# A second attention product on 64x64 tiles in two banks, with the transposes in one of them

## The reference

```python
for c in range(nc):                       # 24 chunks of 32, 4 batches, 8 heads, head size 64
    scores = scale * q_c @ k_full.T       # 32 x 64
    a = np.exp(scores - max);  a = a / (sum(a) + 1e-9)
    out[c] = a @ v_full                   # the second attention product
# x = heads side by side
h = x @ w_in;  e = np.exp(h - max);  solu = h * e / (sum(e) + 1e-9)
ln = (solu - mean) / sqrt(var + 1e-6) * g_ln
y = ln @ w_out                            # 3072 x 512
g = np.maximum(0.01 * (y @ w_in2), y @ w_in2);  out = g @ w_out2
```

## Time and profile before

| | us |
|---|---|
| median of three runs (lowest, highest) | 807.08 (806.21, 808.84) |
| the profiled execution | 806.93 |
| its span, first to last instruction | 805.1 |
| busy: PE, PEld, DVE, ACT, POOL | 793.7, 652.5, 542.0, 454.7, 62.6 |
| mean granted TensorE clock | 0.999 of full speed |
| one `expo`, 128x384 | 0.52 |
| one `rsum`: sum, addition, reciprocal | 0.55, 0.18, 0.19 |
| one `probs` on GpSimd | 0.83 |
| one `x_lo` (xT_lo), 128x384 | 0.55 |
| one `solu`: product, read of the sum, mean | 1.21, 0.08, 0.15 |
| one `expo1`, one `norm`, one `tr`, 128x1024 | 1.11, 1.24, 1.22 |

### The profile page before, as it was taken

The page is one execution under the profiler, slowest core; times in us unless marked ns, Lnnn a source line. Parts: engine busy times, 40 slices in busy tenths (PEclk is TensorE's granted clock), DMA queues, the critical chain, the costliest instruction groups (busy, mean ns, idle before and its releaser), DMA issues.

```text
span 805.1 us, 14444 instructions
## 1 busy us (share of the span) xinstructions
PE 793.7 (99%) x5604; PEld 652.5 (81%) x5604; DVE 542.0 (67%) x902; ACT 454.7 (56%) x737; POOL 62.6 (8%) x156
## 2 busy tenths in 40 slices
PE   8989999999999999999999999999999999999998
PEld 6778888888888888888888888888888888888886
DVE  6788889987632556436652335756799698779774
ACT  5578877777543345256574447666644555445553
POOL 1233332332100000000000000000000000000000
PEclk9999999999999999999999999999999999999999
DMA  9855878755938975167684567545933740462002
GB/s 357 290 173 199 254 242 249 220 163 138 303 93 274 319 270 210 52 209 248 224 285 158 202 234 244 171 166 174 375 135 102 264 158 26 140 245 113 27 1 78
DMA packets 79891, 156.72 MB, mean 195 GB/s; under 512 B 6224, under 2 KB 30928, under 8 KB 79824
## 3 DMA queue, kind: packets, MB, share of 16 engines
q1 hardware_dynamic: 79824, 155.81, 57.4%
HBM read 99.16 MB, written 56.62 MB: 193 GB/s over the span
## 4 chain that ended last, share of the span: by engine, by line
PE 92%; DVE 4%; DMA 2%; issue 1%; ACT 1%; SPq 0%; POOL 0%; DVEq 0%; ACTq 0%
PE hid_a L731 23%; PE hid_b L731 21%; PE scores_ps L731 21%; PE attn_ps L731 13%; PE probs_ps L731 7%; PE attn_ps L723 3%; PE scores_ps L697 2%; DMA g_scratch<-g_out 1%; PE probs_ps L709 1%; DVE ring_lo L1147 1%; DVE g_blk L1289 0%; DMA attn_buf<-qk_in 0%; DVE unit_max L1165 0%; DVE g_blk L1294 0%; DVE shifted L1168 0%
## 5 line engine op out<-in xcount | busy, mean ns | idle before, releaser
L862 ACT ACTIVATE ring_hi<-g_blk 128x512 fp32r<-128x512 f32 x168 | 105.8, 632 | 108.2 <-PE hid_b L731 40.1
L1147 DVE TENSOR_TENSOR ring_lo<-g_blk,ring_hi 128x512 fp32r<-128x512 f32 x168 | 115.6, 688 | 38.4 <-ACT ring_hi L862 35.3
L1011 ACT ACTIVATE g_out<-g_out 128x512 f32<-128x512 f32 x72 | 45.4, 630 | 71.3 <-DVE g_out L1273 41.1
L731 PE MATMUL scores_ps<-x_op_P_hi,w_hi 128*128 128x512 f32 x144 | 56.1, 390 | 0.0
L731 PE MATMUL scores_ps<-x_op_P_lo,w_hi 128*128 128x512 f32 x144 | 56.0, 389 | 0.0
L731 PE MATMUL scores_ps<-x_op_P_hi,w_lo 128*128 128x512 f32 x144 | 56.0, 389 | 0.0
L731 PE MATMUL hid_b<-ring_hi,w_hi 128*128 128x512 f32 x128 | 50.0, 391 | 0.2 <-DVE ring_lo L1147 0.2
L731 PE MATMUL hid_b<-ring_lo,w_hi 128*128 128x512 f32 x128 | 49.9, 390 | 0.0
L731 PE MATMUL hid_b<-ring_hi,w_lo 128*128 128x512 f32 x128 | 49.8, 389 | 0.0
L731 PE MATMUL hid_a<-w_in_hi,xT_hi 128*128 128x512 f32 x96 | 39.6, 412 | 1.0 <-DVE xT_lo L1147 0.9
L1147 DVE TENSOR_TENSOR w_lo<-w_raw,w_hi 128x1792 fp32r<-128x1792 f32 (+2 forms) x24 | 33.6, 1401 | 8.4 <-ACT w_hi L862 8.2
(11 more groups left out here) (178 smaller groups left out, 2043.7 us busy)
## 6 DMA issues: line engine op xcount, KB each, us to landing
g_scratch<-g_out SPq DMA_DIRECT2D x96, 256.0 KB, 2.7
g_blk<-g_scratch SPq DMA_DIRECT2D x48, 512.0 KB, 7.3
attn_buf<-qk_in SPq DMA_DIRECT2D x32, 576.0 KB, 6.5
attn_buf<-v_in SPq DMA_DIRECT2D x32, 384.0 KB, 3.9
ln_scratch<-lnT SPq DMA_DIRECT2D x24, 512.0 KB, 6.3
w_raw<-w_in SPq DMA_DIRECT2D x16, 512.0 KB, 4.4
ln_even<-ln_scratch SPq DMA_DIRECT2D x12, 512.0 KB, 6.6
ln_odd<-ln_scratch SPq DMA_DIRECT2D x12, 512.0 KB, 7.2
```

What stands on the lines that cost most here:

```text
L731: mm = pe.matmul(psum, weights[i], data[j], start=first and n == 0, stop=last and n == 2, skip_group_check=goes_on)
L862: return act.activation(dst, src, ACT.Copy)
L1011: act.activation(x, x, ACT.Prelu, alpha=0.01).then_inc(s_g[q], 1)
L1147: return ve.tensor_tensor(dst, x, hi.bitcast(f32), ALU.subtract)
```

## The change

- `values` becomes 24 products on 64x64 tiles (64 rows by 64 columns of weights, 32 columns of data, straight from the transposed probabilities `prob_t`). The two row halves write to two banks, `attn_ps[:, 0:512]` and `attn_ps[:, 512:]`.
- `spread` becomes one copy of 128x384 from PSUM into `prob_t`; `diag` with its memsets is gone.
- `probs_ps` is gone: the transposes write into the first bank of `attn_ps`. So `probs_t` of a unit waits for `x_lo` of the unit before instead of for `spread`.
- `x_hi` and `x_lo` read the two banks and write every second run of 32 tokens, through a four-dimensional view.
- The list of steps is written anew: `probs_t` and `values` of the same unit now follow each other with one slice of `hidden` between them; in BLOCK_STEPS T of 4t+3, H, V of 4t+3, S of 4t+6. START and TAIL are reordered likewise.

```diff
 START, from its fifth line:
+        ("values", 1), ("load_v", 5), ("probs", 2), ("x_hi", 1), ("x_lo", 1),
+        ("scores", 3), ("load_qk", 7), ("w1_lo", 1),
+        ("hidden", 1, 0), ("shift", 3), ("w1_hi", 2),
+        ("probs_t", 2), ("spread", 2), ("expo", 3),
+        ("hidden", 0, 1), ("w1_lo", 2), ("rsum", 3), ("w1_hi", 3), ("probs", 3),
+        ("values", 2), ("load_v", 6), ("x_hi", 2), ("x_lo", 2),
+        ("hidden", 1, 1), ("w1_lo", 3),
+        ("hidden", 0, 2),
+        ("probs_t", 3), ("spread", 3),
+        ("hidden", 1, 2),
+        ("values", 3), ("load_v", 7), ("x_hi", 3), ("x_lo", 3),
+        ("scores", 4), ("load_qk", 8), ("shift", 4), ("expo", 4), ("rsum", 4), ("probs", 4),
+        ("hidden", 0, 3),
+        ("scores", 5), ("load_qk", 9), ("shift", 5), ("neg_max", 0), ("expo", 5),
+        ("hidden", 1, 3), ("expo1", 0), ("rsum", 5), ("probs", 5),
+        ("probs_t", 4), ("stats_a", 0), ("spread", 4), ("solu", 0),
+        ("scores", 6), ("load_qk", 10), ("square", 0), ("neg_max", 1),
+        ("values", 4), ("load_v", 8), ("stats", 0), ("x_hi", 4), ("x_lo", 4),
+        ("hidden", 2, 0), ("shift", 6), ("expo1", 1), ("expo", 6), ("rsum", 6), ("probs", 6), ("stats_a", 1),
+        ("probs_t", 5), ("spread", 5), ("solu", 1), ("norm", 0),
+        ("hidden", 2, 1), ("square", 1), ("tr", 0),
+        ("values", 5), ("load_v", 9), ("x_hi", 5), ("x_lo", 5),
+        ("scores", 7), ("load_qk", 11), ("shift", 7), ("expo", 7), ("rsum", 7), ("probs", 7),
+        ("hidden", 2, 2),
+        ("scores", 8), ("load_qk", 12), ("shift", 8), ("expo", 8), ("rsum", 8), ("probs", 8),
+        ("probs_t", 6), ("spread", 6),
+        ("values", 6), ("load_v", 10),
 BLOCK_STEPS, its middle:
+        ("probs_t", 4), ("spread", 4), ("norm", -1), ("w1_lo", 2),
+        ("hidden", 0, 3), ("neg_max", 0),
+        ("values", 4), ("load_v", 8), ("x_hi", 4), ("x_lo", 4),
+        ("scores", 7), ("load_qk", 11), ("expo1", 0), ("shift", 7), ("stats_a", 0),
+        ("hidden", 1, 1), ("expo", 7), ("solu", 0),
+        ("hidden", 1, 2), ("rsum", 7), ("probs", 7),
...
 def probs_t(a):
                 if a >= 1:
-                    pe.wait_ge(s_spread, 2 * a)
+                    pe.wait_ge(s_x_lo, a)
...
             def values(a):
                 pe.wait_ge(s_v_in[a % SLOTS], 16 * (a // SLOTS + 1))
-                pe.wait_ge(s_spread, 2 * (a + 1))
-                if a >= 1:
-                    pe.wait_ge(s_x_lo, a)
+                pe.wait_ge(s_spread, a + 1)
+                buf, pt = attn_buf[a % SLOTS], prob_t[a % 2]
+                for pair in range(BLOCK_CHUNKS // 2):
+                    for r in range(2):
+                        rows = slice(ROWS * r, ROWS * r + ROWS)
                         for hb in range(2):
+                            n = 2 * pair + hb
+                            first = BLOCK + SEG + n * HEAD_DIM
+                            mm = pe.matmul(attn_ps[64 * hb:64 * hb + 64, HALF * r + CHUNK * pair:HALF * r + CHUNK * (pair + 1)],
+                                           buf[rows, first:first + HEAD_DIM],
+                                           pt[rows, n * CHUNK:(n + 1) * CHUNK], start=True, stop=True)
                 mm.then_inc(s_values, 1)
...
             def spread(a):
-                for half in range(2):
-                    rows = slice(64 * half, 64 * half + 64)
-                    copy(diag[a % 2][rows, :, half, :],
-                         probs_ps[rows, 0:BLOCK].rearrange("k (n q) -> k n q", q=CHUNK)).then_inc(s_spread, 1)
+                copy(prob_t[a % 2][:, :], attn_ps[:, 0:BLOCK]).then_inc(s_spread, 1)
...
             def x_hi(a):
-                copy(xT[t % 2][0][:, hp, :], attn_ps[:, 0:BLOCK]).then_inc(s_x_hi, 1)
+                copy(of_halves(xT[t % 2][0][:, hp, :]), attn_halves).then_inc(s_x_hi, 1)
...
-            for i in range(2):
-                ve.memset(diag[i][:, :, :, :], 0.0).then_inc(s_init, 1)
```

More of the change, by code:

```diff
@@ L118 @@
         ("hidden", 0, 0), ("expo", 2), ("w1_hi", 1), ("rsum", 2),
[L119 to L143, removed]
@@ L170 @@
-        ("hidden", 2, 2), ("rsum", 8), ("square", 1),
-        ("probs_t", 7),
-        ("values", 6), ("load_v", 10), ("tr", 0), ("probs", 8), ("w1_hi", 3),
+        ("scores", 5), ("load_qk", 9), ("x_hi", 2), ("x_lo", 2), ("stats", -2),
+        ("hidden", -1, 3), ("norm", -2), ("shift", 5),
+        ("hidden", 0, 0), ("expo", 5), ("neg_max", -1), ("rsum", 5), ("probs", 5),
+        ("probs_t", 3), ("spread", 3),
+        ("hidden", 0, 1), ("expo1", -1), ("tr", -2), ("solu", -1), ("stats_a", -1),
@@ new lines @@
+        ("values", 3), ("load_v", 7), ("x_hi", 3), ("x_lo", 3),
+        ("scores", 6), ("load_qk", 10), ("square", -1), ("shift", 6),
+        ("hidden", 0, 2), ("expo", 6), ("stats", -1),
+        ("hidden", 1, 0), ("rsum", 6), ("probs", 6),
+        ("probs_t", 4), ("spread", 4), ("norm", -1), ("w1_lo", 2),
+        ("hidden", 0, 3), ("neg_max", 0),
+        ("values", 4), ("load_v", 8), ("x_hi", 4), ("x_lo", 4),
+        ("scores", 7), ("load_qk", 11), ("expo1", 0), ("shift", 7), ("stats_a", 0),
@@ new lines @@
+        ("hidden", 1, 1), ("expo", 7), ("solu", 0),
+        ("hidden", 1, 2), ("rsum", 7), ("probs", 7),
+        ("probs_t", 5), ("spread", 5), ("square", 0), ("tr", -1),
+        ("hidden", 1, 3), ("neg_max", 1), ("stats", 0),
+        ("values", 5), ("load_v", 9), ("x_hi", 5), ("x_lo", 5),
+        ("scores", 8), ("load_qk", 12), ("norm", 0), ("shift", 8),
+        ("hidden", 2, 0), ("expo1", 1), ("stats_a", 1), ("expo", 8),
+        ("hidden", 2, 1), ("solu", 1),
+        ("probs_t", 6), ("spread", 6), ("square", 1), ("rsum", 8), ("probs", 8),
@@ L173 @@
+        ("hidden", 2, 2), ("tr", 0), ("w1_hi", 3),
+        ("values", 6), ("load_v", 10),
 )
 TAIL = (
-        ("hidden", 20, 3), ("x_hi", 30), ("stats", 19), ("spread", 31), ("x_lo", 30),
+        ("hidden", 20, 3), ("x_hi", 30), ("stats", 19), ("x_lo", 30),
         ("hidden", 21, 0), ("neg_max", 20), ("norm", 19),
+        ("probs_t", 31), ("spread", 31),
         ("hidden", 21, 1), ("expo1", 20), ("tr", 19),
@@ L322, in build @@
     prob = [at(f"prob{i}", (77 + 1.5 * i) * KB, [P, BLOCK]) for i in range(2)]
-    diag = [at(f"diag{i}", (112 + 3 * i) * KB, [P, BLOCK // P * 4, 2, CHUNK]) for i in range(2)]
+    prob_t = [at(f"prob_t{i}", (112 + 1.5 * i) * KB, [P, BLOCK]) for i in range(2)]
     xT = [[at(f"xT{i}_{x}", (place + 6 * j) * KB, [P, KM, BLOCK], f32r) for j, x in enumerate(("hi", "lo"))]
@@ L1183, in x_lo @@
                 ve.wait_ge(s_x_hi, a + 1)
-                rest(xT[t % 2][1][:, hp, :], attn_ps[:, 0:BLOCK], xT[t % 2][0][:, hp, :]).then_inc(s_x_lo, 1)
+                rest(of_halves(xT[t % 2][1][:, hp, :]), attn_halves, of_halves(xT[t % 2][0][:, hp, :])).then_inc(s_x_lo, 1)
             def neg_max_(n):
```

25 lines of the change are left out of this document (8 added, 17 removed).

## The result

The changed kernel takes 821.2 us (median of 4 runs, 820.5 to 825.0) against 806.9 for the kernel before on the same chip: ratio 1.018, 95% interval 1.015 to 1.022. It is slower by 14 us, where 4 were forecast and 816 was the upper end of the range. Its mean granted clock is 0.987; the other three executions show 0.990 to 0.992, so the share of the clock in the sum is that of this execution.

The account below looks back on a forecast made before the run. TensorE, busy 99% of the span, was taken to bound the kernel. Its own work -0.2, regular part +0.3 and START's waits +3.7 gave +3.8 us on 807.1, so 810.9 us; range 808.0 to 816.0.

Parts of the forecast that it names:

- Direction and mechanism: Whole kernel: slower, chance 0.78, with idle time in START before PE steps waiting for spread, x_lo and shift.
- PE's own work, -0.2: TensorE over 32 units: products -0.9 us, starts of four tiles +0.4, transposes and entry to values +0.3; sum -0.2.
- serial loads: Rival, values step: weight loads of two row tiles go one after the other, +19 us, 829 or so; 10%.
- a pace set by the data: Rival, values step: data, not load, sets the pace; 0.36 us, some 800 us total; faster 5%, swallowed by VectorE 5%.
- The estimate of 1.2 us for V: Values step: 48 instructions at 25 ns each by the skill's page, against the forecast's own 0.70 us.
- as laid: Whole kernel: the forecast without its rivals, 809.8 to 813.7 us; 58%.
- Waits of START, +3.7: PE in START: eight waits after the first sum to 10.1 us in the new order against 6.4 before, +3.7.
- T5's and V5's waits: START, unit 5: transposes wait 0.97 us for x_lo 4, values wait 0.32 us for spread 5.
- The clock, a rival at 10% and +3: START: waits of 2.3 and 2.6 us drop TensorE to 1.2 GHz, +3 us, 814 in all; 10%.
- +3.8 whole: Whole kernel: the summed change, counted fully because TensorE has only 4 us idle behind the attention stage.
- The regular part, +0.3: Regular part: only the hidden slice behind solu is late, by 0.1 us in some blocks, +0.3 us.
- So no wait there: Regular part: a hidden slice gives 1.37 us for the 0.49 us spread copy, x_lo has 3.4 us; no wait.

Follow-up runs that it names:

- e_order: The kernel before, with its old products, two diagonal copies and separate banks, given the changed kernel's START, BLOCK_STEPS and TAIL; 821.53 us, ratio 1.018.
- e_sp4: The changed kernel with one step moved: expo1 0 behind spread 4 instead of ahead of it on ScalarE; 820.10 us, ratio 1.0176.
- e_wide: The changed kernel with 64 instead of 32 columns of data in 20 of 24 products of each values step; 820.75 us, ratio 1.017.
- e_pause: The kernel before with five spare 0.48 us copies on ScalarE ahead of the diagonal copies of units 4 and 6; 811.62 us, ratio 1.0055.
- e_fill2: The changed kernel with unused identity products put into START's waits: 8 before values 4, 8 before scores 8, 10 before values 6; 819.24 us, ratio 1.0145.
- e_warm: The changed kernel with the first series of warm-up products 1 instead of 7; 818.16 us, ratio 1.0138.
- e_best1: The changed kernel with searched new orders of both START and BLOCK_STEPS; 810.55 us, ratio 1.0035.
- e_start1: The changed kernel with a searched new order of START alone; 813.34 us, ratio 1.008.

## Why the prediction was wrong

- **Direction and mechanism: right.** Slower, by waits in START where PE reads what spread, x_lo and shift bring. e_order shows that the new order is enough for a loss of this size, though not in the same places, and e_sp4 how a wait goes to the next step.
- **PE's own work, -0.2: right.** V to S 0.83 us, and V's pace is not the data's (e_wide). The rivals of serial loads and of a pace set by the data are out. The estimate of 1.2 us for V that the Trainium skill would give (TensorEngine Tiling (Array Packing), Instruction Overhead) is not borne out: 48 instructions take 0.90 us. (The band "as laid" starts at 809.8, where its lower bound was worked out as 809.5; nothing hangs on it.)
- **Waits of START, +3.7: sized 0.7 short.** They are +4.4. The steps that were laid came within some 0.4 us each; the stop of V0 and S2's late data weren't in the laying-out, and T5's and V5's waits, 1.3 us of it, were hidden by the slow clock.
- **The clock, a rival at 10% and +3: this is the step that failed.** The prediction carried +3.8 whole and left the clock at full, because the earlier trace rows show it unmoved by 1.3 us of idle time. But waits of 2 us and more, close together, lie outside that row. Three stretches at 1.2 GHz cost 6.9 us. e_pause gives the price of one, 2.5 us, behind a wait of 2.2 us in the kernel before; e_fill2 takes two away by filling the waits. The third, at 12.8 us, came behind S2's late data and V0's stop and is gone where both are (e_warm). The clock can't be read from the length of one wait: 1.99 us ahead of V4 lowered it in the changed kernel and not in e_wide. The Trainium skill (TensorE: Matmul & The Clock Gate, Why this matters for your kernels) warns of longer pauses between bursts of products than any single wait in this kernel. Here the clock fell behind waits of 2.0 to 2.2 us, and the measurement decides.
- **The regular part, +0.3: mis-sized, it is +3.9.** "So no wait there" followed the copy from T to V, 0.49 us in a slice of 1.37, but not what stands ahead of spread on ScalarE. norm waits for GpSimd's stats behind probs, and expo1, expo and spread wait with it. With another BLOCK_STEPS the waits are gone (e_best1, 2.8 us under e_start1).

The sum: -0.2 counted in the rest, waits 4.4, clock 6.9, regular part 3.9, less the 0.5 behind V31: 14.7 us, the difference of the spans. The 6.9 are the remainder of the first stretch of that sum, so that it must come out; the count by steps (7.1) is what supports them. The range failed with the clock: its upper end took one fall of the clock, alone.

What is still open is why the transfers of PE's program come no earlier, what besides the length of a wait decides whether the clock falls, why S2's data come late in most of these kernels (0.9 us in the changed one) and not in the one before, and whether the new products would pay with the best order for each.
